# Early loads of q, k and v issued by GpSimd, and bias tiles loaded six supertiles behind their stores

## What is computed

```python
# q, k, v: (4, 8, 576, 64)
x = log1p(|i - j|) / log1p(max(i, 1))                 # 576 x 576, the same for all batches
bias = relu(x[..., None] @ w1 + b1) @ w2              # 32 hidden values, 8 heads
attn = softmax(q @ k.T / 8 + bias)                    # rows of 576
x = (attn @ v) as 2304 x 512
x = max(x @ moe_w1, x @ moe_w2, x @ moe_w3) @ moe_w_out
h = x @ moe2_w_in
out = where(h >= 1, h, where(h <= -1, 0, (h + 1)**2 / 4)) @ moe2_w_out
```

## Time and profile before

| | us |
|---|---|
| median of 3 runs | 1026.89 |
| lowest, highest | 1025.89, 1028.06 |
| the profiled execution | 1028.29 |
| its span, first to last instruction | 1026.5 |
| PE busy | 994.7 (97%) |
| DVE, ACT, POOL busy | 503.6, 490.7, 295.8 |
| mean granted clock of PE | 0.992 |

### The profile page before, as it was taken

How to read it: one execution, slowest core, us unless ns; L and a number is a source line. 1 busy time by engine, 2 the same in 40 slices (tenths; PEclk the granted TensorE clock), 3 DMA queues, 4 the chain that set the end, 5 groups by cost and what they waited for, 6 DMA issues and landing times.

```text
span 1026.5 us, 20413 instructions
## 1 busy us (share of the span) xinstructions
PE 994.7 (97%) x7608; PEld 865.4 (84%) x7608; DVE 503.6 (49%) x1176; ACT 490.7 (48%) x1023; POOL 295.8 (29%) x506
## 2 busy tenths in 40 slices
PE   6959999999999999999999999999999999999998
PEld 3547767776767999999999999889989989899897
DVE  8946667667683231313232327754454444544543
ACT  8948788778783321212121225543343443433433
POOL 1049888888873700000000336700000000000000
PEclk9979999999999999999999999999999999999999
DMA  5872534425312400000000113200000000000000
GB/s 142 265 222 57 151 73 107 124 50 155 93 40 64 131 33 1 1 0 0 0 0 0 42 62 92 94 8 25 1 31 0 0 31 0 31 0 0 32 1 32
DMA packets 96043, 56.10 MB, mean 55 GB/s; under 512 B 64224, under 2 KB 81632, under 8 KB 95968
## 3 DMA queue, kind: packets, MB, share of 16 engines
q1 hardware_dynamic: 95872, 55.11, 19.0%
q10 hardware_dynamic: 96, 0.00, 0.0%
HBM read 39.46 MB, written 15.63 MB: 54 GB/s over the span
## 4 chain that ended last, share of the span: by engine, by line
PE 73%; DVE 1%; issue 0%; POOL 0%; ACT 0%; ACTq 0%; DVEq 0%
PE ps L1078 42%; PE ps L1137 20%; PE ps L1105 7%; PE ps L1029 2%; PE ps L977 1%; PE ps L990 1%; DVE s_sb L796 0%; PE ps L1004 0%; POOL probs L518 0%; PE ps L953 0%; DVE p_t L810 0%; DVE x_lo L851 0%; DVE row_min L796 0%; ACT o_sb L747 0%; DVE xT L817 0%
## 5 line engine op out<-in xcount | busy, mean ns | idle before, releaser
L1078 PE MATMUL ps<-x_hi,w_all 128*128 128x384 f32 x1632 | 437.8, 336 | 1.2 <-ACT ta L693 1.2
L1078 PEld LDWEIGHTS ps<-x_hi,w_all 128*128 128x128 f32 x1632 | 296.8, 188 | 7.2 <-DVE xT L817 1.7
L1078 PE MATMUL ps<-x_lo,w_all 128*128 128x384 f32 x816 | 273.2, 335 | 0.0
L1137 PE MATMUL ps<-w_all,g_hi 128*128 128x512 f32 x576 | 179.9, 393 | 0.0
L1078 PEld LDWEIGHTS ps<-x_lo,w_all 128*128 128x128 f32 x816 | 153.2, 188 | 3.9
L538 POOL TENSOR_TENSOR w_all<-raw,w_all 128x256 fp32r<-128x256 f32 x100 | 77.6, 807 | 273.8 <-ACT w_all L667 273.8
L796 DVE CUSTOM_DVE_ANT_0 s_sb<-ps,bias_h 128x576 f32<-128x576 f32 (+1 forms) x160 | 114.8, 753 | 80.3 <-PE ps L977 55.3
L602 ACT ACTIVATE probs<-s_sb,row_min 128x576 f32<-128x576 f32 (+1 forms) x160 | 122.2, 770 | 6.8 <-DVE row_min L796 6.8
L518 POOL TENSOR_SCALAR probs<-probs,row_inv 128x576 f32<-128x576 f32 (+1 forms) x160 | 121.3, 768 | 13.7 <-DVE row_inv L826 12.6
L1137 PEld LDWEIGHTS ps<-w_all,g_hi 128*128 128x128 f32 x576 | 106.2, 188 | 19.5 <-issue 1.2
L1137 PE MATMUL ps<-w_all,g_lo 128*128 128x512 f32 x288 | 113.9, 395 | 0.0
(11 more groups left out here) (85 smaller groups left out, 1327.4 us busy)
## 6 DMA issues: line engine op xcount, KB each, us to landing
bias_scratch<-p_t SPq DMA_DIRECT2D x36, 296.0 KB, 3.8
raw<-in_moe_w_out SPq DMA_DIRECT2D x22, 256.0 KB, 3.1
bias_h<-bias_scratch SPq DMA_DIRECT2D x16, 288.0 KB, 4.2
raw<-in_moe_w SPq DMA_DIRECT2D x18, 256.0 KB, 3.0
out<-o_sb SPq DMA_DIRECT2D x18, 256.0 KB, 2.1
q_in<-in_q SPq DMA_DIRECT2D x32, 128.0 KB, 2.4
bias_h<-bias_scratch SPq DMA_DIRECT2D x16, 256.0 KB, 3.2
v_in<-in_v SPq DMA_DIRECT2D x32, 128.0 KB, 2.4
```

The lines of the kernel that those rows point to most:

```text
L1078: last = pe.matmul(ps[:, bank, 0:BLK], w[:, at:at + P], x[:, kt, :], start=(kt == 0 and n == 0), stop=(kt == KT - 1 and n == 2))
L1137: last = pe.matmul(ps[:, O_BANK + t, :], g[:, ft % 4, t * P:(t + 1) * P], w[:, wout_d(ft):wout_d(ft) + DM], start=(opens and i == 0), stop ...
```

## The change

The helpers `load_q`, `load_k` and `load_v` take the issuing engine as an argument. POOL issues q and k of pair 1 once 14 copies are done, those of pair 2 once 26 are done (and `lo_ok` has reached 5), and then the first v; they have semaphores of their own (`qk_first`, `v_first`), and PE's waits follow. POOL's slots come after these issues in its program. SP's list of the first part keeps the stores; bias tile 0 follows stores 14 and 15, tile 1 stores 22 and 23, tile 2 stores 30 and 31, each with a wait for the first 8, 16 or 24 stores; tiles 3 and 4 follow the last store.

```diff
--- before.py
+++ after.py
@@ -158,6 +158,8 @@
         bias_free = [sem(f"bias_free{e}") for e in range(NB)]
         bias_in = [[sem(f"bias_in{e}_{t}") for t in range(NT)] for e in range(2)]
         qk_in = [sem(f"qk_in{e}") for e in range(2)]
+        qk_first = {i: sem(f"qk_first{i}") for i in (1, 2)}
+        v_first = sem("v_first")
         vv_in = [sem(f"vv_in{e}") for e in range(2)]
         pads_zero = sem("pads_zero")
         turn_ps, t_ps, t_cp = sem("turn_ps"), sem("t_ps"), sem("t_cp")
@@ -298,6 +300,39 @@
         Y_BANK = 4
         O_BANK = 4
 
+        def load_q(eng, i):
+            par, landed = i % 2, qk_first.get(i, qk_in[i % 2])
+            for h in range(2):
+                x = q[i % B, 2 * (i // B) + h, :, :]
+                eng.dma_start(q_in[:, par, 0:T, h, :],
+                             x[0:MAIN, :].rearrange("(t p) d -> p t d", t=T)).then_inc(landed, 16)
+                eng.dma_start(q_in[0:HALF, par, T, h, :], x[MAIN:S, :]).then_inc(landed, 16)
+
+        def load_k(eng, i):
+
+            par, landed = i % 2, qk_first.get(i, qk_in[i % 2])
+            x = k[i % B, 2 * (i // B), :, :]
+            eng.dma_start(k_in[:, par, 0:T, 0, :],
+                         x[0:MAIN, :].rearrange("(t p) d -> p t d", t=T)).then_inc(landed, 16)
+            eng.dma_start(k_in[0:HALF, par, T, 0, :], x[MAIN:S, :]).then_inc(landed, 16)
+            x = k[i % B, 2 * (i // B) + 1, :, :]
+            halves = x[0:MAIN, :].rearrange("(t r p) d -> r p t d", t=T, r=2)
+            eng.dma_start(k_in[HALF:P, par, 0:T, 1, :], halves[0]).then_inc(landed, 16)
+            eng.dma_start(k_in[0:HALF, par, 1:NT, 1, :], halves[1]).then_inc(landed, 16)
+            eng.dma_start(k_in[0:HALF, par, 0, 1, :], x[MAIN:S, :]).then_inc(landed, 16)
+
+        def load_v(eng, i):
+
+            if i >= 2:
+                eng.wait_ge(o_ps, 2 * (i - 2) + 2)
+            landed = vv_in[i % 2] if i else v_first
+            for h in range(2):
+                x = v[i % B, 2 * (i // B) + h, :, :]
+                eng.dma_start(v_in[:, i % 2, h, 0:T, :],
+                             x[0:MAIN, :].rearrange("(t p) d -> p t d", t=T)).then_inc(landed, 16)
+                eng.dma_start(v_in[h * HALF:(h + 1) * HALF, i % 2, h, T, :],
+                             x[MAIN:S, :]).then_inc(landed, 16)
+
         block = ctx.enter_context(nc.Block())
 
         @block.sync
@@ -317,44 +352,12 @@
                 sp.dma_start(w2b[r * HID:(r + 1) * HID, r * H:(r + 1) * H], w2).then_inc(w2_in, 16)
 
 
-            def load_q(i):
-                par = i % 2
-                for h in range(2):
-                    x = q[i % B, 2 * (i // B) + h, :, :]
-                    sp.dma_start(q_in[:, par, 0:T, h, :],
-                                 x[0:MAIN, :].rearrange("(t p) d -> p t d", t=T)).then_inc(qk_in[par], 16)
-                    sp.dma_start(q_in[0:HALF, par, T, h, :], x[MAIN:S, :]).then_inc(qk_in[par], 16)
-
-            def load_k(i):
-
-                par = i % 2
-                x = k[i % B, 2 * (i // B), :, :]
-                sp.dma_start(k_in[:, par, 0:T, 0, :],
-                             x[0:MAIN, :].rearrange("(t p) d -> p t d", t=T)).then_inc(qk_in[par], 16)
-                sp.dma_start(k_in[0:HALF, par, T, 0, :], x[MAIN:S, :]).then_inc(qk_in[par], 16)
-                x = k[i % B, 2 * (i // B) + 1, :, :]
-                halves = x[0:MAIN, :].rearrange("(t r p) d -> r p t d", t=T, r=2)
-                sp.dma_start(k_in[HALF:P, par, 0:T, 1, :], halves[0]).then_inc(qk_in[par], 16)
-                sp.dma_start(k_in[0:HALF, par, 1:NT, 1, :], halves[1]).then_inc(qk_in[par], 16)
-                sp.dma_start(k_in[0:HALF, par, 0, 1, :], x[MAIN:S, :]).then_inc(qk_in[par], 16)
-
             def load_qk(i):
 
                 if i >= 3:
                     sp.wait_ge(lo_ok, NT * (i - 1))
-                load_q(i)
-                load_k(i)
-
-            def load_v(i):
-
-                if i >= 2:
-                    sp.wait_ge(o_ps, 2 * (i - 2) + 2)
-                for h in range(2):
-                    x = v[i % B, 2 * (i // B) + h, :, :]
-                    sp.dma_start(v_in[:, i % 2, h, 0:T, :],
-                                 x[0:MAIN, :].rearrange("(t p) d -> p t d", t=T)).then_inc(vv_in[i % 2], 16)
-                    sp.dma_start(v_in[h * HALF:(h + 1) * HALF, i % 2, h, T, :],
-                                 x[MAIN:S, :]).then_inc(vv_in[i % 2], 16)
+                load_q(sp, i)
+                load_k(sp, i)
 
             def load_bias(hp, h, t):
 
@@ -385,26 +388,11 @@
 
             for s in range(NSUP):
                 store_bias(s)
-                if s == 8:
-                    load_q(1)
-                if s == 14:
-                    load_k(1)
-                if s == 22:
-                    sp.wait_ge(lo_ok, NT)
-                    load_q(2)
-                if s == 26:
-                    load_k(2)
-                if s in (11, 12):
-                    first_bias(s - 11, 0, s - 3)
-                if s in (NSUP - 3, NSUP - 2):
-                    first_bias(s - NSUP + 3, 1, 2 * P // SUP)
-            for t in range(2, T):
+                if s % 8 in (6, 7) and 14 <= s < NSUP - 4:
+                    first_bias(s % 8 - 6, s // 8 - 1, s // 8 * 8)
+            for t in range(T - 1, NT):
                 for h in range(2):
-                    first_bias(h, t, (t + 1) * P // SUP)
-            sp.wait_ge(staged_zero, 1)
-            load_v(0)
-            for h in range(2):
-                first_bias(h, T, NSUP)
+                    first_bias(h, t, min((t + 1) * P // SUP, NSUP))
 
             def weights(u):
                 e = u % 2
@@ -435,7 +423,7 @@
                 if 1 <= i < GROUPS - 2:
                     load_qk(i + 2)
                 if i:
-                    load_v(i)
+                    load_v(sp, i)
                 if i == GROUPS - 3:
                     weights(0)
                     weights(1)
@@ -539,6 +527,14 @@
                                               w_hi[:, at + c:at + c + PIECE].bitcast(F32), ALU.subtract)
                 last.then_inc(w_ok, 1)
 
+            for i, done in ((1, 14), (2, 26)):
+                pool.wait_ge(bias_sb, done)
+                if i == 2:
+                    pool.wait_ge(lo_ok, NT)
+                load_q(pool, i)
+                load_k(pool, i)
+            pool.wait_ge(staged_zero, 1)
+            load_v(pool, 0)
             for w in range(NU + 1):
                 slot(w)
 
@@ -1004,7 +1000,10 @@
                     last = pe.transpose(ps[:, T_BANK, 0:n], probs[0:n, u % RING, MAIN:MAIN + P], ident[0:n, 0:n])
                 for n, j in enumerate(js):
                     if j % NT == 0:
-                        pe.wait_ge(qk_in[j // NT % 2], 144 * (j // NT // 2 + 1))
+                        if j // NT in qk_first:
+                            pe.wait_ge(qk_first[j // NT], 144)
+                        else:
+                            pe.wait_ge(qk_in[j // NT % 2], 144 * (j // NT // 2))
                     at = 2 * n * P if w < 2 else P
                     turn_in(T_BANK, at, q_in, j // NT % 2, j % NT)
                     last = turn_in(T_BANK, at + P, k_in, j // NT % 2, j % NT)
@@ -1018,7 +1017,10 @@
                 if units[0] == 0:
                     tiles = (2, NT)[half]
                     if half == 0:
-                        pe.wait_ge(vv_in[i % 2], 64 * (i // 2 + 1))
+                        if i == 0:
+                            pe.wait_ge(v_first, 64)
+                        else:
+                            pe.wait_ge(vv_in[i % 2], 64 * ((i + 1) // 2))
                     pe.wait_ge(p_cx, NT * i + tiles)
                     pe.wait_ge(p_cy, T * i + min(tiles, T))
                     pe.wait_ge(t_cp, NT * i + tiles + LAG)
```

## The result

The changed kernel takes 1031.46 us (median of 7 runs, 1029.87 to 1032.08), the kernel before 1028.00 beside it (7 runs, 1025.89 to 1029.23): ratio 1.003, 95% interval 1.0021 to 1.004. The forecast was 1020.7, so the direction is wrong. The profiled execution took 1029.87 us, its span is 1028.0, which is 1.5 more than before; it is the shortest of the seven.

What follows compares the result with a forecast made beforehand. Bias tiles late in SP's lagging queue were taken to stall DVE and PE after the bias stage. 8.1 - 0.2 - 1.7 = 6.2 us off 1026.9 gave 1020.7 us; range 1018.6 to 1037.

Steps and rivals of the forecast that it cites:

- part 3: Bias stage: 22 load issues on POOL at 1.0 us each, done by 56 us, hidden in idle time at no cost.
- the bounds, 0.68 and 2.4 us per issue: POOL's price per issue: lower bound from SP's issues of k, upper from the time such a load takes to land.
- The slower rival: POOL's issues are slow beside DVE, so POOL is late for its slot 0; at 2.4 us each, 1035 us; chance 0.34.
- Part 1: Bias tiles 0 to 2 moved forward in SP's queue, no wait added, so slot 1's DVE work needs only scores.
- the sum's first term: Gain from the earlier bias tiles: slot 5 at 68.9 instead of 77.05 us, 8.1 us at most.
- No stall of over 2 us would remain to bring it down: PE's low clock at the early slots would go with the long stall; its gain is included in the 8.1 us.
- Part 2: Taking 22 issues off SP gives back its 7 us lag, so stores follow ACT's copies.
- Traffic: DMA traffic after 28 us delays bias tile 4: between nothing and 2.0 us lost, 1.7 taken.
- POOL disturbing DVE: POOL's issues slow DVE's bias-stage instructions: taken as 0, up to 6.3 us for 18 issues kept for the range.
- POOL's own pace: POOL's slots 1 to 4 fall behind PE's earlier slots; slack of 2.0 us leaves 0.2 us lost.

Runs made afterwards that it cites:

- tiles_only: Kernel before with only bias tiles 0, 1 and 2 moved to their new places, all q, k, v loads left on SP; 1027.36 us, ratio 0.9994.
- sp_early_only: Changed kernel with all q, k and v loads on SP, issued early, and none on POOL; 1024.31 us, ratio 0.9962 to the kernel before.
- pool_start_12: Changed kernel with POOL's loads of both pairs started at copy 12 instead of 14 and 26; 1023.97 us, ratio 0.9967 to the kernel before.
- pool_start_13: Changed kernel with POOL's loads of both pairs started at copy 13 instead of 14 and 26; 1030.59 us, ratio 1.0031 to the kernel before.
- two_breaks: Changed kernel with two added DVE pauses, before supertiles 16 and 28; 1027.24 us, ratio 1.0001 to the kernel before.
- pair2_v_at_12: Changed kernel with pair 1 on SP behind stores 3 and 6, POOL issuing pair 2 and v at copy 12; 1024.05 us, ratio 0.9963.
- pool_at_start: Changed kernel with pair 1 and v issued by POOL at program start, pair 2 on SP behind stores 11 and 15; 1025.15 us, ratio 0.9978.

## Why the prediction was wrong

**The step that failed** is in part 3: "I take 1.0 us, near SP's rows since it is the same transfer that is described, and POOL is done at 43 + 13 = 56: it costs nothing, hidden in 54 us of idle time." An issue on POOL isn't the same work as one on SP: SP's issues of the same loads pass beside the same DVE stream (0.43 to 1.65 us in tiles_only and sp_early_only), POOL's are held as its writes are. The 21 that came after the stream cost less than 1.0 us, the one within it 25.68. Its price is no price per issue at all but the distance to DVE's next pause, and the cover that was to hide it, DVE's unbroken stream to 54 us, is what makes it. So neither of the bounds, 0.68 and 2.4 us per issue, held the truth (the argument that SP never paid over 0.9 was misread besides: 0.88 is the mean of k's five, and one of them took 1.63): times from rows of a queue that DVE doesn't hold up can't bound one that it does. POOL was done at 67.5 instead of 56. The direction follows: late pair 1 puts a bubble of 8.69 us where one of 6.37 had been.

**The slower rival** had the right mechanism, POOL's issues slow beside DVE, and the wrong shape: 13 issues at 2.4 us and 1035. The decisive load was not the last in line, whose end at 58.98 the rival watched, but the first, pair 1, which the prediction gave 14.7 us and did not look at again. The Trainium skill, SBUF — State Buffer, section "SBUF: two separate sides", describes a lock: whichever of the two engines starts first, DVE with an instruction in a two-port mode, has the shared port for the whole instruction, and a DMA of GpSimd's is blocked until DVE's instruction ends and some 115 ns more. The runs agree that DVE's form decides (two sources: 0.98 us) and that the release follows DVE's end closely (0.3 us). They differ in the length: not one instruction of 0.5 us but the whole unbroken run of them, up to 26.87 us. By its 3100 ns per DMA every issue beside DVE would have been slow; in pool_start_12 all 22 passed beside it, none over 1.02 us.

**Part 1 and the sum's first term** hold where POOL gets through. From slot 0 to slot 5 pool_start_12 takes 15.3 us, against 21.8 before and the 13.7 (68.9 less 55.2) of the forecast. What is missing, 1.6 us, is slots 2 and 3 at the clock of 1.2 GHz (0.74 + 0.82 over 2.74; the granted clock is 0.50 from 62 to 67 us). "No stall of over 2 us would remain to bring it down" was true of the stalls, 1.45 us at most, and false of the clock. The shift reached the end whole: slot 5 5.1 us earlier, span 1021.0 against 1026.5.

**Part 2** was right, SP's 7 us went (store 27 at 46.2). That the tiles need SP freed first, tiles_only shows: no gain without it.

**What was given back.** Traffic was put at 1.7 us; in pool_start_12 DVE waits for no bias tile between 57 and 74 us, so it is nothing there, though the DMA engines are at 0.97 to 1.00 from 28 to 60; where SP issues everything DVE waits 2.75 us for one tile and 1.3 more for two others. POOL disturbing DVE was taken as 0 with 6.3 as the bound: 22 issues beside DVE put slot 0 at 56.63, 1.4 us later than the 55.21 of before, and 13 at the start cost DVE about 1.6. It belonged in the sum, near its lower end. POOL's own pace, put at 0.2, does not show. With 8.1 less 1.6 for the clock and 1.4 for DVE the sum is 5.1, slot 5's shift in pool_start_12; its medians differ by 4.0 (1027.98 and 1023.97), a difference between executions that the profile of one doesn't show.

**The size of the loss.** The profiled execution explains 1.5 of the 3.5 us between the medians. The rest fits what pool_start_13, with the same held issue, shows in an execution of 1031.36 us: there four slots in a row run at 0.61 (slots 1 to 4), where the changed kernel's has two, slot 5 comes at 80.40, and the span is 3.0 over that of before. For the changed kernel itself only one execution was profiled, so this is likely, not shown.

**The range** from 1018.6 to 1037.0 holds 1031.5 through the slower rival, whose chance had been 0.34.

## What to carry to other kernels

In this kernel moving DMAs to GpSimd's queue was cheap only where the first of them began in a break of DVE's one-source stream, or close to one. Before such a move, look for DVE instructions with one SBUF source that run without a pause, and put the issues before them, into a pause, or on another queue; even then one of a series can be caught. An idle engine is not a cover: ask what its instruction shares with the engine that is busy. And where a transfer is moved, price the one that is wanted first behind it (here pair 1), not only the last.

## What the runs showed of the hardware that was not expected

- A DMA issue on GpSimd beside DVE's one-source SBUF stream is held until DVE's next pause (idle, or an instruction from PSUM): 25.68 us from 28.51, 26.87 from 27.30, 18.55 from 36.18, 10.98 from 43.28, 4.18 to a pause put there on purpose. DVE loses nothing meanwhile.
- It isn't held if it starts in a pause (0.98 us at 29.37), just before one (22.48) or soon after DVE's stream was broken (26.31), nor at the program's start (4.7); those behind it pass at 0.54 to 1.02 us, with one exception in the runs (21.70 us from 33.28). Such passing issues slow DVE's blocks, by 1.6 us for 13 of them (pool_at_start) and 1.4 for 22 (pool_start_12).
- A memset of one column is held in the same way (25.64 us).
- The same load costs GpSimd 0.55 us (64 partitions' tail) and 0.80 (the main part) to issue, against 0.43 to 1.65 on SP (tiles_only, sp_early_only).
- PE's granted clock was 0.50, the level of 1.2 GHz, at slots 2 and 3 of pool_start_12 (62 to 67 us) though PE had not been idle for over 1.5 us at a stretch; it did so in slot 3 of two_breaks and not before slot 5 of pair2_v_at_12, so where it falls isn't given by the longest stall alone.
